# Attention rewritten inside a fused attention and mixture-of-experts kernel: split operands for the scores, scores joined by a predicated copy, row sums from a column of ones

## The reference

```
scores = (q @ k^T) / 8                    # 4 batches x 8 heads, 768 positions, head size 64
keep   = (key < n_sink) or (0 <= query - key < window)     # n_sink 4, window 128
a      = softmax(where(keep, scores, -1e9)) ; x = a @ v
h      = x @ w_in ;  y = (h * cos(h)) @ w_out              # 3072 x 512, hidden 2048
# then each token goes to the best of 8 experts (512 -> 1024 -> 512, relu), scaled by its gate
```

## Time and profile before

| | us |
|---|---|
| median of 3 runs | 1146.75 |
| lowest, highest run | 1143.53, 1148.73 |
| the profiled execution | 1143.03 |
| its span | 1141.4 |
| stage 1, first score matmul to first matmul of stage 2 | 10.4 to 258.95 |
| mean granted TensorE clock | 0.995 |

### The profile page before, as it was taken

How to read it: one execution, slowest core, us unless ns; L and a number is a source line. 1 busy time by engine, 2 the same in 40 slices (tenths; PEclk the granted TensorE clock), 3 DMA queues, 4 the chain that set the end, 5 groups by cost and what they waited for, 6 DMA issues and landing times.

```text
span 1141.4 us, 20256 instructions
## 1 busy us (share of the span) xinstructions
PE 1105.1 (97%) x6312; PEld 921.4 (81%) x6313; DVE 720.7 (63%) x1892; ACT 489.6 (43%) x1087; POOL 134.9 (12%) x251
## 2 busy tenths in 40 slices
PE   5999999999999999999999999999999999999997
PEld 4777777777888888888888887888888999899996
DVE  6888888984447866865875876886743222522225
ACT  4777777774334334334333334334442212421114
POOL 0000000001000000000000000240231222222213
PEclk9999999999999999999999999999999999999999
DMA  4444445534002001001100200102362111411102
GB/s 126 146 126 138 133 133 149 149 125 180 1 1 74 1 1 56 19 1 38 37 1 1 74 1 1 40 22 75 113 220 94 46 46 38 154 61 45 54 19 93
DMA packets 35725, 80.77 MB, mean 71 GB/s; under 512 B 11342, under 2 KB 11726, under 8 KB 35536
## 3 DMA queue, kind: packets, MB, share of 16 engines
q1 hardware_dynamic: 29456, 65.60, 18.3%
q0 software_dynamic: 6208, 14.40, 3.8%
HBM read 60.90 MB, written 21.69 MB: 72 GB/s over the span
## 4 chain that ended last, share of the span: by engine, by line
PE 86%; DMA 4%; DVE 3%; issue 3%; SPq 3%; ACT 1%; DVEq 0%; POOL 0%; POOLq 0%; ACTq 0%
PE bank L1528 24%; PE bank L1542 23%; PE bank L1614 13%; PE bank L1629 12%; PE bank L1403 5%; DMA v_sink<-v_n 3%; PE bank L1437 2%; PE bank L1448 2%; PE bank L1415 2%; PE bank L1580 1%; SPq L424 1%; PE bank L1405 1%; SPq L416 1%; DVE masked L951 1%; SPq L419 0%
## 5 line engine op out<-in xcount | busy, mean ns | idle before, releaser
L1528 PE MATMUL bank<-x_hi,w_hi 128*128 128x512 f32 x384 | 153.3, 399 | 2.6 <-DVE g_sb L1117 2.0
L1528 PE MATMUL bank<-x_hi,w_lo 128*128 128x512 f32 x384 | 152.6, 397 | 0.0
L1528 PE MATMUL bank<-x_lo,w_hi 128*128 128x512 f32 x384 | 152.4, 397 | 0.0
L1542 PE MATMUL bank<-w_hi,g_hi 128*128 128x512 f32 x384 | 151.8, 395 | 0.5 <-DVE g_lo L1122 0.5
L1542 PE MATMUL bank<-w_hi,g_lo 128*128 128x512 f32 x384 | 152.0, 396 | 0.0
L1542 PE MATMUL bank<-w_lo,g_hi 128*128 128x512 f32 x384 | 151.9, 396 | 0.0
L1326 DVE SCALAR_TENSOR_TENSOR g_lo<-bank,g_hi 128x256 fp32r<-128x256 f32 x112 | 47.4, 424 | 162.3 <-ACT g_hi L839 162.2
L1403 PE MATMUL bank<-k_sb,qz 128*128 128x256 f32 (+1 forms) x384 | 115.7, 402 | 18.7 <-issue 10.4
L1614 PE MATMUL bank<-xg_hi,w_hi 128*128 128x256 f32 x448 | 126.3, 282 | 2.4 <-issue 2.4
L1614 PE MATMUL bank<-xg_lo,w_hi 128*128 128x256 f32 x448 | 125.8, 281 | 0.0
L1614 PE MATMUL bank<-xg_hi,w_lo 128*128 128x256 f32 x448 | 125.5, 280 | 0.0
(11 more groups left out here) (188 smaller groups left out, 2178.9 us busy)
## 6 DMA issues: line engine op xcount, KB each, us to landing
raw<-w_expert SPq DMA_DIRECT2D x32, 512.0 KB, 5.0
raw<-w_dense SPq DMA_DIRECT2D x16, 512.0 KB, 5.2
k_sb<-k_t SPq DMA_DIRECT2D x16, 384.0 KB, 3.3
qz<-q_t SPq DMA_DIRECT2D x32, 192.0 KB, 4.0
v_sb<-v_n SPq DMA_DIRECT2D x16, 384.0 KB, 4.3
xT_scratch<-x_stage SPq DMA_DIRECT2D x16, 384.0 KB, 5.4
x_raw<-xT_scratch SPq DMA_DIRECT2D x6, 1024.0 KB, 5.2
y_scratch<-y_sb SPq DMA_DIRECT2D x6, 1024.0 KB, 4.4
```

The source lines that it names most:

```text
L1528: last = pe.matmul(H_BANK[f % 2][:, :], a[:, w], b[:, k, :], start=x == 0, stop=x == 3 * KD - 1)
L1542: last = pe.matmul(Y_BANK[t][:, :], a[n % 3][:, t * P:(t + 1) * P], b[:, w], start=f == 0 and x == 0, stop=f == FB1 - 1 and x == 2)
```

## The change

Only the attention path for a small window and the splitting of weights are rewritten.

- The host now lays q out twice, on rows 0 to 63 and again on rows 64 to 127 of a tile for each head, and k likewise, with the 32 sink keys inserted after every even block of keys. ScalarE rounds q (times -0.125) and k into `qs` and `k_hi` in eight parts a pair (`split_part`); GpSimd makes the rests (`part_rest`): rows 64 to 127 of `qs` become the rest of q, and `k_lo` the rest of k. For the first pair VectorE does it (`first_rests`).
- The scores of a head are two fp32r matmuls of 288 columns (160 in a pair's first step), with `k_hi` and with `k_lo`, over 128 rows; a third matmul of 32 columns adds a large number to the sink columns that are masked.
- In a block of 128 keys of the window, each query keeps a key either of the previous or of the own block at the same position. A predicated copy puts the two together (`join_scores`), 2x128 elements for both heads, and a reduction takes the extremes of 2x160. The mask is gone, and so is the padding of q. The window must now be exactly 128.
- The exponentials read PSUM and write 160 columns a head, the two heads interleaved. Two blocks a step are transposed instead of four, and the sinks of two steps as one block straight from the probabilities. The copy from PSUM multiplies the block with two triangles, which yields both blocks of keys again.
- The product with v has the probabilities as 128 columns of weights and 65 columns of v and ones as moving data, so that the row sums come with it. The sinks are one matmul of 260 columns for two steps. VectorE scales the result (`scale_o`), TensorE transposes it (`turn_o`), and ScalarE copies it to `x_stage`.
- Stage 1 splits only the weights `w_in`, half a piece a pair. The 8 pieces of `w_out` are split in slices 0 to 7 of stage 2's first chunk (`split_later`), and `down` of that chunk waits for them.
- Score buffers are two pairs of PSUM banks; the transposes have one bank instead of two.

The lines that the change takes out are those of the functions shown above; of the diff, these are the lines put in, with the lines around them where they say more:

```diff
+    WIDE = P + SINK
+    KW = S + QB // 2 * SINK
+    CUT = S // 2, QB // 2 * P + 2 * SINK
     GROUPS = QB // 2
...
+    VW = P + 2
+    UNSEEN = 1.0e30
+    HIDDEN = 8589934592.0
     xT_dram = nc.dram_tensor("xT_scratch", (KD, P, N), F32).ap()
...
+        twin = [ctx.enter_context(nc.psum_tensor(f"twin{i}", [P, 2, 512], F32)) for i in range(2)]
+        bank = [twin[i // 2][:, i % 2, :] for i in range(4)]
+        bank += [ctx.enter_context(nc.psum_tensor(f"bank{i}", [P, 512], F32)) for i in range(4, 8)]
         wg_sb = sb("wg_sb", [P, KD, NE])
...
+        def group(it, m):
+            return STEPS // 2 * it + m // 2
+        def part(c):
+            half, h, is_k = c // 4, c % 4 // 2, c % 2
+            cut_at = CUT[is_k]
+            return is_k, h, slice(half * cut_at, cut_at if half == 0 else (KW if is_k else S))
...
+        JOINED = slice(P, P + WIDE)
+        def probs_of(m, h, at=0, count=WIDE):
+            start = 2 * WIDE * (m % 2) + 2 * at + h
+            return probs[:, m // 2 % 2, start:start + 2 * count - 1:2]
+        def block_of(m, h):
+            return probs_of(m, h, SINK if m % 2 else 0, P)
...
+        PIECE_STEP = 3
         HALF = PIECE // 2
...
+        TURN_LAG, PV_LAG, SCALE_LAG, STAGE_LAG = 2, 3, 4, 5
+        T_BANK, O_BANK, X_BANK = bank[4], bank[5:7], bank[7]
...
+            def load_part(pair, c):
+                is_k, h, cols = part(c)
+                to, of, width = (raw_k, k_twice, KW) if is_k else (raw_q, q_twice, S)
+                sp.dma_start(to[:, h, cols], of[bass.ds(pair, 1), :, h * width + cols.start:h * width + cols.stop].rearrange("o p s -> (o p) s"),
+                             ).then_inc(qk_loaded[c], 16)
+            def load_parts(it, i, cs):
+                for c in cs:
+                    sp.wait_ge(part_lo_made, 8 * (2 * it + i + 1) + c + 1)
+                    load_part(2 * it + i + 2, c)
+            def load_v(it, i):
+                at_least(sp, sinks_weighed, GROUPS * (2 * it + i - 1))
                 pair = 2 * it + i
...
                 if isinstance(it, int) and it == 0:
...
+                    sp.wait_ge(rows_cleared, 3 * (i + 1))
+                sp.dma_start(v_sb[i][:, :, 1:P + 1],
+                             v[bass.ds(pair, 1), :, :].rearrange("o p (b s) -> (o p) b s", s=P)).then_inc(v_loaded[i], 16)
                 for u in range(4):
...
+                    at = VW * (u // 2) + (1 if u % 2 == 0 else HD + 1)
+                    sp.dma_start(v_sink[i][HD * (u // 2) + u % 2:HD * (u // 2 + 1):2, at:at + HD],
                                  v[bass.ds(pair, 1), 0:SINK, HD * (u % 2):HD * (u % 2 + 1)].rearrange("o p s -> (o p) s"),
...
+                                 ).then_inc(v_loaded[i], 16)
...
+                def during_pair(it, i, last=False):
+                    if not last:
+                        load_parts(it, i, range(0, 3))
+                    if not (last and i == 1):
+                        load_v(*after_pair(it, i))
+                    if not last:
+                        load_parts(it, i, range(3, 5))
+                    if i == 1:
+                        store_pair(it, 0)
+                    elif not (isinstance(it, int) and it == 0):
+                        store_pair(it - 1, 1)
+                    if not last:
+                        load_parts(it, i, range(5, 8))
+                        load_piece(it + 1, i)
+                for c in range(8):
...
+            def part_rest(it, i, c):
+                is_k, h, cols = part(c)
+                pool.wait_ge(part_hi_made, 8 * (2 * it + i) + c + 1)
+                pool.wait_ge(part_lo_made, 8 * (2 * it + i) + c)
+                at_least(pool, w_lo_made, 2 * it + i - (1 if c < 5 else 0))
                 pool.sem_inc(carried_pool, 1)
...
+                if is_k:
+                    pool.tensor_tensor(k_lo[i][:, h, cols], raw_k[:, h, cols], k_hi[i][:, h, cols].bitcast(F32), ALU.subtract).then_inc(part_lo_made, 1)
+                else:
+                    pool.tensor_scalar(raw_q[HD:, h, cols], raw_q[HD:, h, cols], -0.125, None, ALU.mult).then_inc(q_scaled, 1)
+                    pool.wait_ge(q_scaled, 4 * (2 * it + i) - 4 + c // 2 + 1)
+                    pool.sem_inc(carried_pool, 1)
+                    pool.tensor_tensor(qs[i][HD:, h, cols], raw_q[HD:, h, cols], qs[i][HD:, h, cols].bitcast(F32), ALU.subtract).then_inc(part_lo_made, 1)
+            def piece_rest(it, i, last):
+                pool.wait_ge(w_hi_made, 2 * it + i + 1)
+                if not last:
+                    pool.wait_ge(part_lo_made, 8 * (2 * it + i + 1) + 5)
+                pool.sem_inc(carried_pool, 1)
+                dst = bass.ds((2 * it + i) * HALF, HALF)
+                pool.tensor_tensor(w_lo[:, dst], raw[:, i, 0:HALF], w_hi[:, dst].bitcast(F32), ALU.subtract).then_inc(w_lo_made, 1)
+            def rests(it, last=False):
+                for n in range(STEPS):
+                    if not (last and n >= QB):
+                        for c in PARTS[n % QB]:
+                            part_rest(*after_pair(it, n // QB), c)
...
+            def split_part(it, i, c):
+                is_k, h, cols = part(c)
+                act.wait_ge(qk_loaded[c], 16 * (2 * it + i) + 16)
+                if is_k:
+                    act.activation(k_hi[i][:, h, cols], raw_k[:, h, cols], ACT.Copy).then_inc(part_hi_made, 1)
+                else:
+                    act.activation(qs[i][:, h, cols], raw_q[:, h, cols], ACT.Copy, scale=-0.125).then_inc(part_hi_made, 1)
...
             def exponentials(it, n):
...
+                act.wait_ge(max_made, STEPS * it + n + 1)
+                at = lagged(it, n, 4)
+                if at:
+                    act.wait_ge(probs_turned, STEPS * at[0] + at[1] + 1)
+                    act.wait_ge(sinks_turned, group(*at) + 1)
                 for h in range(2):
...
+                    act.activation(probs_of(n, h), twin[n % 2][:, h, JOINED], ACT.Exp, scale=-1.0,
+                                   bias=neg_max[:, 2 * n + h:2 * n + h + 1]).then_inc(probs_made, 1)
...
+            def copy_sinks(it, m):
+                g = group(it, m)
+                act.wait_ge(sinks_turned, g + 1)
+                at_least(act, sinks_weighed, g)
+                act.activation(sink_probsT[:, :], X_BANK[:, 2 * P:3 * P], ACT.Copy).then_inc(sinksT_made, 1)
...
+            def split_later(f):
+                act.wait_ge(later_loaded[(f + 2) % 4], 16 * (f // 4) + 16)
+                act.activation(w_hi[:, (EP + f) * PIECE:(EP + f + 1) * PIECE], raw[:, (f + 2) % 4, :], ACT.Copy).then_inc(later_hi_made, 1)
...
+            def split_later(f):
+                dve.wait_ge(later_hi_made, f + 1)
+                dst = slice((EP + f) * PIECE, (EP + f + 1) * PIECE)
+                dve.tensor_tensor(w_lo[:, dst], raw[:, (f + 2) % 4, :], w_hi[:, dst].bitcast(F32), ALU.subtract).then_inc(later_lo_made, 1)
...
+            def join_scores(it, n):
+                i, both = n % QB, [P, 2, P]
+                to = twin[n % 2]
+                dve.wait_ge(scores_done, STEPS * it + n + 1)
+                dve.sem_inc(carried_dve, 1)
+                own = slice(WIDE, WIDE + P) if i % 2 else slice(P, 2 * P)
+                from_block = to[:, :, 0:P] if i else unseen[:, :].unsqueeze(1).broadcast_to(both)
+                dve.copy_predicated(to[:, :, own], prior[:, :].bitcast(U32).unsqueeze(1).broadcast_to(both), from_block).then_inc(scores_joined, 1)
+                dve.wait_ge(scores_joined, STEPS * it + n + 1)
+                dve.tensor_reduce(neg_max[:, 2 * n:2 * n + 2], to[:, :, JOINED], AX.X, ALU.min).then_inc(max_made, 1)
             def copy_probs(it, m):
...
+                first = 1 if m % QB == 0 else 0
+                shape = [P, 2 - first, 2, P]
                 dve.wait_ge(probs_turned, STEPS * it + m + 1)
                 at_least(dve, window_weighed, STEPS * it + m - 1)
...
+                turned = T_BANK[:, 0:2 * P].rearrange("p (h q) -> p h q", h=2)
+                dve.tensor_tensor(probsT[m % 2][:, first:, :, :], turned.unsqueeze(1).broadcast_to(shape),
+                                  halves_of[:, first:, :].unsqueeze(2).broadcast_to(shape), ALU.mult).then_inc(probsT_made, 1)
...
+            def scale_o(it, m):
+                g, slot, shape = group(it, m), m // 2, [P, 2, 2, HD]
+                o = O_BANK[slot % 2][:, 0:2 * VW].rearrange("p (b w) -> p b w", b=2)
+                dve.wait_ge(sinks_weighed, g + 1)
+                dve.tensor_scalar(den[:, slot, :, :], o[:, :, 0:VW:P + 1], 1e-9, None, ALU.add).then_inc(den_made, 1)
+                dve.wait_ge(den_made, g + 1)
+                dve.reciprocal(rden[:, slot, :, :], den[:, slot, :, :]).then_inc(rden_made, 1)
+                dve.wait_ge(rden_made, g + 1)
+                at_least(dve, o_turned, g)
+                dve.tensor_tensor(o_sb[:, :, :].rearrange("p b (h d) -> p b h d", h=2), o[:, :, 1:P + 1].rearrange("p b (h d) -> p b h d", h=2),
```

(60 more changed lines are left out.)

427 lines of the change are left out of this document (181 added, 246 removed).

## The result

The changed kernel takes 1181.22 us, median of 4 runs (1178.80 to 1183.45), against 1147.05 us for the kernel before on the same chip: ratio 1.0302, interval 1.0268 to 1.0335. It is slower, by 34 us; the prediction was 1121.5 us and faster. The profiled execution took 1182.43 us, 39.4 more than that of before.

A forecast was written before the change was run, and what follows sets the result against it. TensorE was taken as the bound: 12.55 us of passes plus 0.95 of waiting, 13.5 a pair against 15.25. 1143.0 - 28 + 3 = 1118.0 us profiled, 1121.5 as median; range 1107 to 1139.

The forecast's parts named there:

- GpSimd, the step that failed: Stage 1's rests and scaling of q on GpSimd: 10.2 us a pair, hidden under 13.5.
- two streams, 1.8 and 0.9: GpSimd's price in ns an element: 1.8 for two-input subtraction, 0.9 for scaling.
- rival 2: GpSimd becomes the bound; slower if its work exceeds 15.1 us a pair; at 16.6, 1171 us; chance 0.12.
- the upper bound of three streams, 15.0: GpSimd's highest price: subtraction 2.7 and scaling 1.8 ns an element, 15.0 us a pair, giving 1146 us.
- The prediction's 11.7 by the page: GpSimd's work a pair estimated from the skill page's two-input add: near 11.7 us, hidden too.
- ScalarE's 11.4 us: ScalarE's exponentials, splits and copies in stage 1: 11.4 us of a 13.5 us pair, hidden.
- The loop without GpSimd: Stage 1's pair: 12.55 us of TensorE passes plus 0.95 for meshing with VectorE, 13.5 us.
- Rivals 1, 3 and 4: VectorE bounds, 1134 us, 0.22; short v passes unhidden or gaps remain, 1136 to 1148, 0.10; prices too high, 1104, 0.06.
- the wait for v: First scores' wait for the sink rows of v, 0.57 us a pair before, goes through earlier loads.
- The start: Before the first join: plus 1.5 us for VectorE's masks and rests, plus 1 for TensorE's slow first passes.
- The end: Last scores to first dense matmul: 6.5 to 7 us against 6.95; plus 0.5 for the later output.
- Stage 2: Splitting w_out in the first chunk lies in idle time, at zero; without that cover 10 us.

The follow-up runs named there:

- e3: Changed kernel with GpSimd's rests and scalings of q and k cut to 32 columns a part from pair 3 on (scores wrong): 1147.26 us.
- e7: e3 with ScalarE's copy of the turned output moved right behind the exponentials, ahead of the splits: 1138.99 us.
- e12: e1 with ScalarE's copy of the turned output moved right behind the exponentials: 1143.74 us.
- e10: Changed kernel, q's scaling replaced by a scale column in ScalarE's splits, k's rest on 64 rows, output copy right behind the exponentials: 1136.23 us.
- e14: e10 with ScalarE's copy of the turned output at its old place, behind the splits: 1172.12 us.
- e13: e10 with SyncE's first loads for stage 2 (1 MB) issued after the second pair's parts: 1130.60 us.
- e5: Kernel before, with the wait for v moved from a pair's first scores to its first product with v: 1146.13 us, ratio 0.9955.
- e1: Changed kernel with the scaling of q's rows 64 to 127 moved from GpSimd to ScalarE: 1181.88 us.
- e9: Changed kernel with q split unscaled, VectorE multiplying the maximum by -0.125, and the output copy right behind the exponentials: 1176.58 us.
- e11: e9 with the maximum written to a spare column of the scores' PSUM banks and read there: 1144.79 us.
- e6: Changed kernel with ScalarE's copy of the turned output moved right behind the exponentials: 1180.79 us.

## Why the prediction was wrong

Against its 1118.0 us for the profiled execution, the kernel took 1182.4. By its own steps:

- **GpSimd, the step that failed.** The prediction took 10.2 us a pair, "two streams, 1.8 and 0.9" ns an element, and called it hidden. It measured 16.88 us. All three terms were too small. The subtractions take 9.7 us a pair instead of 6.8, at 2.5 to 2.6 ns an element (384 in 1001, 448 in 1140, 512 in 1284) and not 1.8. The scalings, with one input, take 4.7 instead of 1.4, at 3.0 (384 in 1169) and not 0.9. The gaps of 0.17 to 0.3 us between instructions that wait for each other come to 2.5, where 2.0 of overhead was put. So the threshold that rival 2 named, 15.1 us, was passed; its 16.6 a pair and 1171 us were nearly right, at a chance of 0.12. The choice of value had nothing near to rest on: the only rows were a memset and a small copy, one stream each, and the upper bound of three streams, 15.0, was itself below the truth. 14 x (16.74 - 13.5) = 45 us of the miss of 64; of these 45, 31 went with GpSimd's parts cut short (14.50 us a pair, e3). The Trainium skill, "GPSIMD Engine Reference", section "Elementwise, side-by-side cycle accounting", gives 4497 ns for a two-input add of 2048 elements, 2.2 ns an element. The traces agree once a fixed part is taken off: the q rest takes 251 ns for 32 columns (e7) and 1001 for 384, so 2.13 ns an element and 0.18 us fixed, an estimate that comes to 4.55 us at 2048. The prediction's 11.7 by the page is 5.2 us too small: 3.3 of it for the scaling, 1.4 for the subtractions and 0.5 for the gaps.
- **Why the expected gain did not come back at once.** Behind GpSimd stood a second queue. The prediction called ScalarE's 11.4 us "hidden" by its sum and did not ask what stands behind what in its order: a copy that TensorE needs, behind splits that nobody needs yet. e7 prices it at 0.9 us a pair, e12 at 2.6, and e10 against e14 at 2.4.
- **The loop without GpSimd: the total right, in part by luck.** 13.5 us a pair was forecast for TensorE, VectorE and ScalarE together, as 12.55 of TensorE's passes and 0.95 of waiting; with GpSimd and the copy out of the way it is 13.61. But there TensorE is busy for 13.3 us a pair and idle for 0.3 (ten pairs of e7):

```profile
79.22:215.27 136.05, 133.07 (x1072) 128.92 (x1072) 112.34 (x282) 95.56 (x260) 44.48 (x131) 1.00 0.68 202
```

  The sum of passes was too low, mostly in the transposes: the two of a step take 0.32 us (154.47 to 154.79 above) and not 0.21, 0.6 a pair. The waiting was put too high, and the two nearly cancel. The other prices (0.37 a head, 0.84 for the product with v, 0.49 for the sinks, VectorE's predicated copy of 0.428 and reduction of 0.491 us) were forecast at 0.37, 0.85, 0.44, 0.42 and 0.49. Rivals 1, 3 and 4 did not occur, and the wait for v is gone.
- **The start, too small.** Put at +2.5, the two parts of it at 1.5 and 1. VectorE's first join is at 16.79 us instead of 12.56: 4.2. The first pair then takes 18.5 us (14.60 to 33.10), 5 more than forecast; e13 shows such a first pair at 13.35 with the transfers in another order. Nobody had asked what the second pair's q stood behind in SyncE's queue.
- **The end, too small.** Put at +0.5. From the last scores (284.08) to the first dense matmul are 9.1 us, against 6.95; in the last pair itself the scores wait for GpSimd twice, 0.94 and 1.83 us, and the granted clock is 0.68 from 275 to 284 us. With all of this the stretch from the last pair's start to stage 2 is some 9 us of the miss.
- **Stage 2, right; stage 3, +5.1 us, not foreseen.** From the first dense matmul on, TensorE is busy for 339.09 of 341.05 us, before for 339.02. In stage 3 stands one gap ahead of the first passes of L1733 that no semaphore explains (waits of TensorE, the changed kernel from 1100 us on; then the kernel before):

```profile
PE twin L1733 <- issue: 4.1, 1, 4.1
```

```profile
PE bank L1614 <- issue: 0.6, 1, 0.6
```

It is there at 3.5 to 4.1 us in every variant of the changed kernel; in the kernel before and in e5 the longest such gap is 0.6 and 1.9 us. So it goes with the rewritten program and not with the pace of stage 1. Its cause was not tried and stays open, and so does the rest of the 5.1.

## What to carry to other kernels

Work given to an idle engine has to be priced with an instruction of that very kind on that engine; without a row, this case's rows give GpSimd's f32 elementwise work at 384 to 512 columns 2.5 to 3 ns an element, plus about 0.2 us between dependent instructions, and the range should go to that. When relief of the bounding engine gives nothing, look for the wait that took its place before giving up the theory: here two queues could hold the loop, and the edits that gave 0 and 9 us alone gave 45 together. Order an in-order engine by who waits for the result, and a DMA queue likewise: moving one copy, without less work on any engine, was worth 8 us (e3 to e7), 36 (e14 to e10) and 38 (e1 to e12) once GpSimd was relieved, and moving one megabyte 6.

## What the hardware showed that was not expected

- GpSimd's multiply with one input is dearer than its subtraction with two: 1169 against 1001 ns for 64x384. And 64 rows cost as much as 128: the k rests of 448 columns take 1140 ns on 128 rows and 1137 on 64 (e10).
- A VectorE instruction of two elements a row took 716 ns on average beside a busy GpSimd, and 159 with its input in PSUM (e9, e11). It goes the other way too: a weight rest on GpSimd that began just behind VectorE's predicated copy took 1.43 to 1.47 us instead of 1.28 (e6). That is rare: the q rest's mean stays at 1000 to 1002 ns in all these runs.
- Waits of TensorE can cost more than their length: in e14 the same wait of 1.05 us left the clock as it was in some pairs and was followed by a stretch at 1.2 GHz in three, which took 2.3 us longer.
